# Mixing stage: the next tile turned between theta's products, gates and splits reordered, and unread products at the stage's start

## The chip, the cores and the metric

The kernel runs on one core of a Trainium2 chip as one program. The metric is the device time of one execution in microseconds (us). The profile is that of one further execution, taken by the hardware profiler; its span runs from the first to the last recorded instruction. PE is TensorE (PEld its weight loads), DVE is VectorE, ACT is ScalarE, POOL is GpSimd, SP issues the DMAs of the hardware queue.

## The reference

Three stages follow one another: attention restricted to buckets, a mixture of experts with one expert per token, and a token-mixing layer. The change lies in the last one alone:

```python
theta = x @ w_theta                      # x: 2 x 768 tokens, 512 wide
zr, zi = x * np.cos(theta), x * np.sin(theta)
y = np.einsum('ts,bsd->btd', w_tok_r, zr) + np.einsum('ts,bsd->btd', w_tok_i, zi)
u = x + y
out = u + np.maximum(u @ w_ch, 0.0)
```

Here x is the output of the experts, scaled for each token by the probability of its expert (the gate).

## The kernel before

The mixing stage (function `mixing`) works on NC = 12 tiles of 128 tokens (T = 6 for each of two batches), each 512 wide. It starts when the experts' stage has ended on all engines, since its tiles are gathered from what the experts wrote to DRAM. Each engine has a program of its own, written out by hand, and the programs meet at semaphores. An engine works through its program strictly in order, so an instruction that waits holds everything written behind it.

For tile c the steps are these.

- POOL's `gather(c)` issues an indirect DMA that brings the rows of the tile into `x_tok` (semaphore `s_g[c]`).
- `gated(c)` multiplies the tile by its gate, in place: tiles 0 to 2 on DVE (line 1332), the others on ACT (line 1257). The gates are chained by `s_gated`: gate c follows gate c-1.
- PE's `turn_x(c)` transposes the tile into the PSUM tile `m_tp` with four products by an identity (line 1424).
- ACT's `x_high(c)` rounds it to `m_xt_hi` (line 1245), and DVE's `x_low(c)` subtracts that from the unrounded one to give `m_xt_lo` (line 1328). All products are made of three such parts: high by high, high by low, low by high.
- PE's `angles(c)` makes theta for the tile in 12 products of 128x512 (line 1435).
- ACT's `turn(c)` (line 1277) and DVE's `reduce_angle(c)` (four operations, lines 1347 to 1357) bring the angle into the range of the sine.
- ACT's `waves(c)` takes sine and cosine (lines 1283 to 1286), and POOL's `times_x(c)` multiplies them by the tile (two products, line 1227).
- ACT's `z_high(c)` and DVE's `z_low(c)` split the two results. `turn(c)` waits for `z_low(c-2)`, whose buffer it writes.

The token weights come in 12 columns of 768 KB. SP loads column i into `wt_raw` (for i = 1, 3, 5 into `w_raw`), ACT's `columns_high(i)` and DVE's `columns_low(i)` split it into `wt_hi` and `wt_lo`, and PE's `from_tile(n, s)` makes six products of column n and tile s into the PSUM tile `y` (line 1454). SP loads a buffer anew only when `columns_low` has read it.

PE's order is: theta of tiles 0 to 3, with the turns between them; then, step by step, a turn, theta of one more tile, and the products of output tiles 0 to 2 with the tiles that are ready; then output tile 3 (`tokens(3)`), theta of tile 11, output tiles 4 to 6; and at last the product by `w_ch` (`channels(n)`) between the remaining output tiles.

Two earlier stages already hold products that nothing reads: 72 of 128x128 bf16 by an identity `ident_b` at the end of routing (line 848), and 20 at the experts' start (line 1064).

Of the kernel before, what the change touches and what calls it, by code (L numbers as in the profile page):

```python
# [6 lines left out]
BF16 = mybir.dt.bfloat16  # L7
# [6 lines left out]
P = 128  # L14
# [16 lines left out]
NC = B * T  # L31
# [567 lines left out]
KD = DM // P  # L599
# [513 lines left out]
    sp.dma_start(w_raw[:], src.rearrange("(k p) n -> p k n", p=P)).then_inc(s_wraw, 16)  # L1113


def mixing(nc, ctx, w_raw, s_wraw, w_tok, w_ch, y_slots, ident, pos, gate, out):
    def sb(name, shape, dt=F32):
        return ctx.enter_context(nc.sbuf_tensor(name, shape, dt))

# [122 lines left out]
    @block.scalar  # L1242
    def _(act):
        def high(dst, src, done):
            nc.scalar.copy(dst, src).then_inc(done, 1)  # L1245

        def columns_high(i):
            n, raw = raw_of(i)
            act.wait_ge(s_wt[n], landed(i))
            if i >= 3:  # L1250
                act.wait_ge(s_y, i - 2)
            high(wt_hi[i % 3][:], raw, s_wth)

        def gated(c):
            act.wait_ge(s_g[c], 16)
            act.wait_ge(s_gated, c)
            nc.scalar.activation(x_tok[:, c, :], x_tok[:, c, :], ACT.Copy, scale=gate[:, c:c + 1]).then_inc(s_gated, 1)

        def x_high(k):
            act.wait_ge(s_tp, k + 1)  # L1260
            if 2 <= k < NC + 2:
                act.wait_ge(s_th, k - 1)
            elif k >= NC + 2:
                act.wait_ge(s_ch, k - NC - 1)
            high(xt_hi[k % 2][:], tp[k % 2][:], s_xh)

        def z_high(c):
            for at, m in enumerate((1, 0)):
                act.wait_ge(s_z, 2 * c + at + 1)
                high(z_hi[:, c, m, :], z[m][c % 2][:], s_zh)  # L1270

        def turn(c):
            q = c % 2
            act.wait_ge(s_th, c + 1)
            if c >= 2:
                act.wait_ge(s_zl, 2 * c - 2)
            nc.scalar.activation(z[0][q][:], theta[q][:], ACT.Identity, bias=rounder[:],  # L1277
                                 scale=0.15915494309189535).then_inc(s_turn, 1)

        def waves(c):  # L1280
            q = c % 2
            act.wait_ge(s_r, 4 * c + 4)
            nc.scalar.activation(z[1][q][:], angle[q][:], ACT.Sin).then_inc(s_sin, 1)  # L1283
            nc.scalar.activation(z[0][q][:], angle[q][:], ACT.Abs).then_inc(s_sin, 1)
            act.wait_ge(s_sin, 3 * c + 2)
            nc.scalar.activation(z[0][q][:], z[0][q][:], ACT.Sin, bias=half_pi[:], scale=-1.0).then_inc(s_sin, 1)

        act.wait_ge(s_wraw, 16)
        for half in range(2):
            high(wm_hi[:, 2 * half:2 * half + 2, :], w_raw[:, 2 * half:2 * half + 2, :], s_whi)  # L1290
        act.wait_ge(s_c, 2)
        nc.scalar.activation(sine[:], half_pi[:], ACT.Sin).then_inc(s_sine, 1)
        x_high(0)
        columns_high(0)
        for c in range(NC):
            if c + 1 < NC:
                x_high(c + 1)
            if c >= 2:
                z_high(c - 2)
            if c == 0:  # L1300
                columns_high(1)
            turn(c)
            if c + 3 < NC:
                gated(c + 3)
            if c >= 1:
                waves(c - 1)
            if c == 1:
                columns_high(2)
            if c >= 9:
                columns_high(c - 6)  # L1310
        z_high(NC - 2)
        waves(NC - 1)
        columns_high(6)
        z_high(NC - 1)
        act.wait_ge(s_wraw, 32)
        act.wait_ge(s_th, NC)
        high(wm_hi[:], w_raw[:], s_whi)
        for i in (7, 8, 9):
            columns_high(i)
        for n in range(NC):  # L1320
            x_high(NC + n)
            if n in (1, 3):
                columns_high(10 + n // 2)

    @block.vector
    def _(dve):
# [36 lines left out]
        def columns_low(i):  # L1363
            dve.wait_ge(s_wth, i + 1)
            low(wt_lo[i % 3][:], raw_of(i)[1], wt_hi[i % 3][:], s_wtl)
# [12 lines left out]
        gated(0)  # L1378
        x_low(0)
        gated(1)  # L1380
        columns_low(0)
        gated(2)
        for c in range(NC):
            if c + 1 < NC:
                x_low(c + 1)
            if c >= 9:
                add_x(c - 9)
            if c == 1:
                columns_low(1)
            if c >= 2:  # L1390
                z_low(c - 2)
            reduce_angle(c)
            if c == 2:
                columns_low(2)
            if c >= 9:
                columns_low(c - 6)
        z_low(NC - 2)
# [20 lines left out]
    @block.tensor  # L1418
    def _(pe):
        PARTS = ((0, 0), (0, 1), (1, 0))  # L1420

        def transpose(src, k):
            for d in range(KD):
                last = nc.tensor.transpose(tp[k % 2][:, d * P:(d + 1) * P], src[:, d * P:(d + 1) * P], ident[:])  # L1424
            last.then_inc(s_tp, 1)

        def turn_x(c):
            pe.wait_ge(s_gated, c + 1)
            transpose(x_tok[:, c, :], c)

        def project(dst, k, done):
            pe.wait_ge(s_xl, k + 1)
            for d in range(KD):
                for n, (a, w) in enumerate(PARTS):
                    last = nc.tensor.matmul(dst[:], (xt_hi, xt_lo)[a][k % 2][:, d * P:(d + 1) * P],  # L1435
                                            (wm_hi, wm_lo)[w][:, d, :], start=d == 0 and n == 0,
                                            stop=d == KD - 1 and n == 2)
            last.then_inc(done, 1)

        def angles(c):  # L1440
            if c == 0:
                pe.wait_ge(s_wlo, 2)
            if c >= 2:
                pe.wait_ge(s_r, 4 * c - 4)
            project(theta[c % 2], c, s_th)

        def from_tile(n, s):

            c = n // T * T + s
            for m in (1, 0):  # L1450
                if n % T == 0:
                    pe.wait_ge(s_zl, 2 * c + 2 - m)
                for k, (a, w) in enumerate(PARTS):
                    last = nc.tensor.matmul(y[n % 4][:], (wt_hi, wt_lo)[a][n % 3][:, m, s, :],  # L1454
                                            (z_hi, z_lo)[w][:, c, m, :], start=s == 0 and m == 1 and k == 0,
                                            stop=s == T - 1 and m == 0 and k == 2)
            if s == T - 1:
                last.then_inc(s_y, 1)

        def tokens(n):  # L1460
            columns_done(pe, n)
            if n >= 4:
                pe.wait_ge(s_u, n - 3)
            for s in range(T):
                from_tile(n, s)

        def turn_u(n):
            pe.wait_ge(s_u, n + 1)
            transpose(x_tok[:, n, :], NC + n)

        def channels(n):
            if n == 0:
                pe.wait_ge(s_wlo, 3)
                pe.wait_ge(s_r, 4 * NC)
            if n >= 2:
                pe.wait_ge(s_o, n - 1)
            project(ch[n % 2], NC + n, s_ch)

        turn_x(0)
        angles(0)  # L1480
        turn_x(1)
        turn_x(2)
        angles(1)
        turn_x(3)
        angles(2)
        turn_x(4)
        angles(3)

        for s in range(T + 2):
            for n in range(3):  # L1490
                if s == n:
                    columns_done(pe, n)
                if 0 <= s - n < T:
                    from_tile(n, s - n)
            if s + 4 < NC - 1:
                turn_x(s + 5)
                angles(s + 4)
        tokens(3)
        angles(NC - 1)
        tokens(4)  # L1500
        tokens(5)
        tokens(6)
        turn_u(0)
        turn_u(1)
        tokens(7)
        for n in range(NC):
            channels(n)
            if n + 2 < NC:
                turn_u(n + 2)
            if n % 2 == 1 and n < 8:  # L1510
                tokens(8 + n // 2)


def build(nc, qT, kT, v, proj, w_gate, w_local, w1, w2, w_theta, w_tok, w_ch, out):
# [3 lines left out]
    with ExitStack() as whole:  # L1518
        def sb(name, shape, dt=F32):
            return whole.enter_context(nc.sbuf_tensor(name, shape, dt))  # L1520

        ident = sb("ident", [P, P])
        pos = sb("pos", [P, NC], U32)
        gate = sb("gate", [P, NC])
        chunk_tab = sb("chunk_tab", [P, 2, E], I32)
# [4 lines left out]
        with ExitStack() as tokens:  # L1530
# [2 lines left out]
            zeros = routed.enter_context(nc.sbuf_tensor("zeros", [P, DM], F32, side="right"))  # L1533
            x_in = tokens.enter_context(nc.sbuf_tensor("x_in", [P, 2, DM], F32))
            first = tokens.enter_context(nc.sbuf_tensor("first", [P, GATHERED], U32))
            ident_b = tokens.enter_context(nc.sbuf_tensor("ident_b", [P, P], BF16))
            s_first = tokens.enter_context(nc.semaphore("s_first"))
            s_xin0 = [tokens.enter_context(nc.semaphore(f"s_xin0{j}")) for j in range(2)]
            s_rows = tokens.enter_context(nc.semaphore("s_rows"))
# [29 lines left out]
                experts(nc, ctx, w1, w2, x_all, x_rows, x_in, s_xin0, first, s_first, y_out, pos, x_slots, s_clear, y_slots, ident, ident_b, chunk_tab, weights,  # L1569
                        lambda sp: load_w(sp, w_raw, s_wraw, w_theta))  # L1570
        with ExitStack() as ctx:
            mixing(nc, ctx, w_raw, s_wraw, w_tok, w_ch, y_slots, ident, pos, gate, out)


# [31 lines left out]
```

## Time and profile before

| what | value |
|---|---|
| time, median of 3 runs | 684.49 us (684.07, 684.49 and 687.66) |
| time of the profiled execution | 687.27 us |
| its span | 685.4 us |
| PE busy | 632.1 us (92%) |
| DVE busy | 401.0 us (59%) |
| ACT busy | 356.1 us (52%) |
| POOL busy | 250.0 us (36%) |
| mean granted TensorE clock | 0.968 of full speed |

The profiled execution took 1.9 us more than its span. Each run's time is that of the whole program; a granted clock of 1.00 is 2.4 GHz and one of 0.50 is 1.2 GHz. In the mixing stage all times below count from the start of the span; the stage begins at about 488 us.

### The profile page before, as it was taken

The numbers are of one execution on the slowest core, as the hardware profiler recorded it, in microseconds if no ns is written. First come the engines' busy times: TensorE is split into PE (matmuls) and PEld (weight loads), VectorE is DVE, ScalarE is ACT, GpSimd is POOL, SyncE is SP. The second block draws the span as 40 slices with busy tenths as digits, with TensorE's granted clock in tenths as the row PEclk, the third lists the DMA queues.
The fourth block names the chain that finished last, engine by engine and source line by source line (L and its number), as shares of the span: only waits on it lengthen the run. The fifth ranks groups of instructions, "written<-read, shape, count | busy, mean of one in ns | idle before, by whom it ended". The sixth has DMA issues, their size and how long they took to land. (4 is left out here: it accounts for less than half of the span.)

```text
span 685.4 us, 10625 instructions
## 1 busy us (share of the span) xinstructions
PE 632.1 (92%) x3781; PEld 501.6 (73%) x3782; DVE 401.0 (59%) x730; ACT 356.1 (52%) x534; POOL 250.0 (36%) x205
## 2 busy tenths in 40 slices
PE   3899999999999996699999999989479999999998
PEld 1666667767666664598899889979357888878886
DVE  6767777777877754774454344421378777732422
ACT  3776776776776772553365345421266775430200
POOL 5752708163452000287652464250335442200000
PEclk8899999999999999699999999999789999999999
DMA  9203351708163603797976676510462002422201
GB/s 292 92 1 95 144 177 62 254 8 262 39 224 112 227 11 88 264 374 261 364 263 216 231 233 202 179 63 1 157 218 87 17 1 93 153 93 55 85 31 61
DMA packets 57280, 99.24 MB, mean 145 GB/s; under 512 B 17040, under 2 KB 23184, under 8 KB 57232
## 3 DMA queue, kind: packets, MB, share of 16 engines
q1 hardware_dynamic: 54704, 90.47, 39.1%
q0 software_dynamic: 2240, 7.34, 3.0%
q10 hardware_dynamic: 288, 0.79, 0.3%
q8 instruction: 30, 0.49, 0.3%
q14 instruction: 18, 0.15, 0.1%
HBM read 69.23 MB, written 29.36 MB: 144 GB/s over the span
## 5 line engine op out<-in xcount | busy, mean ns | idle before, releaser
L396 DVE TENSOR_REDUCE scores<-scores 128x1 f32<-128x768 f32 x96 | 92.8, 966 | 41.9 <-PE scores L514 40.5
L337 ACT COPY probs_t<-turned 128x768 f32<-128x768 f32 x96 | 76.8, 800 | 63.2 <-PE turned L523 62.9
L345 ACT ACTIVATE probs<-scores,bias,scale 128x768 f32<-128x768 f32 x96 | 95.4, 993 | 12.8 <-DVE bias L403 12.4
L958 POOL TENSOR_TENSOR w_lo<-stage,w_hi 128x1024 fp32r<-128x1024 f32 x28 | 77.4, 2795 | 66.0 <-ACT w_hi L953 63.0
L523 PE MATMUL turned<-ident,probs 128*128 128x128 f32 x576 | 80.4, 276 | 5.0 <-ACT probs_t L337 5.0
L523 PEld LDWEIGHTS turned<-ident,probs 128*128 128x128 f32 x576 | 67.9, 142 | 14.2 <-issue 11.5
L1079 PE MATMUL up<-xt_hi,w_hi 128*128 128x256 f32 x256 | 73.4, 287 | 4.7 <-issue 3.2
L1079 PE MATMUL up<-xt_lo,w_hi 128*128 128x256 f32 x256 | 73.0, 285 | 0.0
L1079 PE MATMUL up<-xt_hi,w_lo 128*128 128x256 f32 x256 | 73.0, 285 | 0.0
L535 PE MATMUL pv<-probs_t,v_in 128*64 128x384 f32 x384 | 72.1, 498 | 0.0
L514 PE MATMUL scores<-k_aug,q_aug 76*128 76x384 f32 x192 | 59.8, 393 | 8.0 <-DVE k_aug L389 5.6
L514 PEld LDWEIGHTS scores<-k_aug,q_aug 76*128 76x128 f32 x192 | 29.3, 193 | 46.2 <-issue 35.3
L953 ACT CAST w_hi<-stage 128x1024 fp32r<-128x1024 f32 x56 | 56.3, 1046 | 4.2 <-DMA stage<-in_w 4.2
L1003 ACT ACTIVATE ht_hi<-up 128x512 fp32r<-128x512 f32 x32 | 19.1, 597 | 74.1 <-PE up L1079 74.1
L1454 PE MATMUL y<-z_hi,wt_hi 128*128 128x512 f32 x144 | 56.7, 394 | 0.0
L1454 PE MATMUL y<-z_lo,wt_hi 128*128 128x512 f32 x144 | 56.2, 391 | 0.0
L1454 PE MATMUL y<-z_hi,wt_lo 128*128 128x512 f32 x144 | 56.1, 390 | 0.0
L1079 PEld LDWEIGHTS up<-xt_hi,w_hi 128*128 128x128 f32 x256 | 49.1, 192 | 5.9 <-issue 4.1
L1095 PE MATMUL down<-w_hi,ht_hi 128*128 128x512 f32 x128 | 51.0, 399 | 0.0
L1032 DVE SCALAR_TENSOR_TENSOR ht_lo<-up,ht_hi 128x512 fp32r<-128x512 f32 x32 | 22.1, 691 | 48.8 <-ACT ht_hi L1003 48.8
L514 PE MATMUL scores<-k_lh,q_hl 128*128 128x384 f32 x192 | 50.5, 344 | 0.0
L1227 POOL TENSOR_TENSOR z<-z,x_tok 128x512 f32<-128x512 f32 x24 | 32.7, 1384 | 48.6 <-ACT z L1283 48.6
(185 smaller groups left out, 1282.5 us busy)
## 6 DMA issues: line engine op xcount, KB each, us to landing
stage<-in_w SPq DMA_DIRECT2D x64, 512.0 KB, 4.7
x_slots<-zeros SPq DMA_DIRECT2D x7, 1024.0 KB, 8.4
y_slots<-zeros SPq DMA_DIRECT2D x7, 1024.0 KB, 10.3
wt_raw<-in_w_tok SPq DMA_DIRECT2D x9, 768.0 KB, 4.4
q_raw<-in_qT SPq DMA_DIRECT2D x16, 384.0 KB, 5.4
k_raw<-in_kT SPq DMA_DIRECT2D x14, 384.0 KB, 6.1
x_in<-x_slots SPq DMA_DIRECT2D x8, 512.0 KB, 6.0
y_slots<-y_out SPq DMA_DIRECT2D x16, 256.0 KB, 4.9
```

The source lines that it names most:

```text
L337: nc.scalar.copy(probs_t[j % 2][:, a, :, t % 3 * P:(t % 3 + 1) * P].rearrange("k (b n) q -> k b n q", b=2), turned[:, :, 0:HALF].rearrange ...
L345: nc.scalar.activation(probs[g % 3][:].rearrange("p (b n) -> p b n", b=2), scores[g % 2][:, :, 0:HALF], ACT.Exp, bias=bias[:, pair, a, t:t ...
L396: nc.vector.tensor_reduce(neg_max[g % 2], scores[g % 2][:, :, 0:HALF], AX.XY, ALU.max, negate=True).then_inc(s_neg, 1)
L514: last = nc.tensor.matmul(scores[g % 2][:, half, 0:HALF], qq[:, rows], kk[:, half * HALF:half * HALF + HALF], start=n == 0, stop=n == 1)
L523: last = nc.tensor.transpose(turned[:, k // 3, k % 3 * P:(k % 3 + 1) * P], probs[g % 3][:, k * P:(k + 1) * P], ident[:])
L535: last = nc.tensor.matmul(pv[a * D:(a + 1) * D, 0:HALF], v_in[pair % 2][:, a, k, :], probs_t[j % 2][:, a, k, :], start=k == 0, stop=k == T ...
L953: nc.scalar.copy(w_hi[w][:, r, :], stage[:, r, :]).then_inc(s_wh, 1)
L958: name.tensor_tensor(w_lo[w][:, r, :], stage[:, r, :], w_hi[w][:, r, :].bitcast(F32), ALU.subtract).then_inc(done, 1)
L1079: last = nc.tensor.matmul(up[f // 2][:, f % 2, :], (w_hi, w_lo)[b][w][:, k, f * P:(f + 1) * P], (xt_hi, xt_lo)[a][:, k, :], start=k == 0 a ...
L1095: last = nc.tensor.matmul(down[j][:], (ht_hi, ht_lo)[a][:, f, j * P:(j + 1) * P], (w_hi, w_lo)[b][w][:, NP // 2 + f // 2, (f % 2) * DM:(f ...
L1227: nc.gpsimd.tensor_tensor(z[m][c % 2][:], z[m][c % 2][:], x_tok[:, c, :], ALU.mult).then_inc(s_z, 1)
L1454: last = nc.tensor.matmul(y[n % 4][:], (wt_hi, wt_lo)[a][n % 3][:, m, s, :], (z_hi, z_lo)[w][:, c, m, :], start=s == 0 and m == 1 and k == ...
```

## The change

In ACT's program `gated(3)` and `x_high(1)` go ahead of everything that concerns columns. Inside the loop `x_high(c+2)` stands behind `turn(c)`, where `x_high(c+1)` stood ahead of it; `gated(c+4)` stands behind `waves(c-1)`, where `gated(c+3)` stood ahead of it. `columns_high(0)` stands behind `turn(0)`, and `columns_high(1)` and `(2)` at the end of c = 1 and 2. DVE's program follows: `gated(2)` and `x_low(1)` ahead of the loop, `x_low(c+2)` behind `reduce_angle(c)`, and `columns_low(0)`, `(1)`, `(2)` at the end of c = 1, 2, 3. In PE's program `turn_x(c+1)` stands amid the 12 products of `angles(c)` for c = 0 to 3. PE's program begins with 48 unread 128x128 bf16 products and has 16 more between `turn_x(0)` and `angles(0)`; `ident_b` is kept until the kernel's end for them. The arithmetic that is read is the same.

```diff
@@ mixing, ACT @@
         x_high(0)
-        columns_high(0)
+        gated(3)
+        x_high(1)
         for c in range(NC):
-            if c + 1 < NC:
-                x_high(c + 1)
             if c >= 2:
                 z_high(c - 2)
+            turn(c)
             if c == 0:
-                columns_high(1)
-            turn(c)
-            if c + 3 < NC:
-                gated(c + 3)
+                columns_high(0)
+            if c + 2 < NC:
+                x_high(c + 2)
             if c >= 1:
                 waves(c - 1)
-            if c == 1:
-                columns_high(2)
+            if c + 4 < NC:
+                gated(c + 4)
+            if c in (1, 2):
+                columns_high(c)
             if c >= 9:
                 columns_high(c - 6)
@@ mixing, DVE @@
         gated(0)
         x_low(0)
         gated(1)
-        columns_low(0)
         gated(2)
+        x_low(1)
         for c in range(NC):
-            if c + 1 < NC:
-                x_low(c + 1)
             if c >= 9:
                 add_x(c - 9)
-            if c == 1:
-                columns_low(1)
             if c >= 2:
                 z_low(c - 2)
             reduce_angle(c)
-            if c == 2:
-                columns_low(2)
+            if c + 2 < NC:
+                x_low(c + 2)
+            if c in (1, 2, 3):
+                columns_low(c - 1)
             if c >= 9:
                 columns_low(c - 6)
@@ mixing, PE @@
-        def project(dst, k, done):
+        def project(dst, k, done, between=None):
             pe.wait_ge(s_xl, k + 1)
             for d in range(KD):
+                if d == KD // 2 and between is not None:
+                    between()
...
+        def keep_clock(times):
+            for n in range(times):
+                nc.tensor.matmul(y[3][:, 0:P], ident_b[:], ident_b[:], start=True, stop=True)
+
+        keep_clock(48)
         turn_x(0)
-        angles(0)
-        turn_x(1)
-        turn_x(2)
-        angles(1)
-        turn_x(3)
-        angles(2)
-        turn_x(4)
-        angles(3)
+        keep_clock(16)
+
+        for c in range(4):
+            angles(c, lambda: turn_x(c + 1))
```

## Rows read from the trace of the kernel before

**Rows 1.** Busy time by stretch: engines (instructions), granted clock, DMA share, GB/s.

```profile
492.00:521.36 29.36, 21.19 (x79) 16.14 (x79) 20.66 (x26) 16.41 (x24) 14.77 (x12) 0.79 0.51 179
521.36:600.00 78.64, 78.64 (x358) 65.12 (x359) 57.89 (x77) 50.84 (x78) 29.18 (x23) 1.00 0.22 74
```

**Rows 2.** Chain that ended last, a piece of it: start, us, what.

```profile
603.60 4.18 DMA wt_raw<-in_w_tok
```

**Rows 3.** Timeline of PE: start, us, line, operands [idle before <-releaser].

```profile
280.73 6.73 PE L848 MATMUL banks<-ident_b 128*128 128x128 bf16 x72
...
459.37 0.38 PE L1079 MATMUL up<-xt_hi,w_hi 128*128 128x256 f32 x1 [1.81 <-issue]
...
492.77 1.12 PE L1424 MATMUL m_tp<-ident,x_tok 128*128 128x128 f32 x4 [8.22 <-DVE x_tok L1332]
495.38 0.77 PE L1435 MATMUL theta<-wm_hi,m_xt_hi 128*128 128x512 f32 x1 [1.49 <-DVE m_xt_lo L1328]
...
500.64 0.85 PE L1424 MATMUL m_tp<-ident,x_tok 128*128 128x128 f32 x4
...
502.89 0.50 PE L1435 MATMUL theta<-wm_hi,m_xt_hi 128*128 128x512 f32 x1 [0.42 <-DVE m_xt_lo L1328]
...
521.36 0.47 PE L1435 MATMUL theta<-wm_hi,m_xt_hi 128*128 128x512 f32 x1 [1.60 <-DVE m_xt_lo L1328]
...
561.93 0.60 PE L1424 MATMUL m_tp<-ident,x_tok 128*128 128x128 f32 x4
...
566.50 0.39 PE L1454 MATMUL y<-z_hi,wt_hi 128*128 128x512 f32 x1
```

**Rows 4.** Short stretches where PE's granted clock changes or holds, columns as in rows 1.

```profile
463.50:464.00 0.50, 0.50 (x6) 0.50 (x5) 0.00 (x0) 0.00 (x0) 0.00 (x0) 0.90 0.00 0
...
487.50:488.00 0.50, 0.00 (x0) 0.00 (x0) 0.00 (x0) 0.00 (x0) 0.00 (x0) 0.50 0.00 0
...
501.00:501.50 0.50, 0.49 (x4) 0.25 (x2) 0.50 (x2) 0.00 (x0) 0.00 (x0) 0.85 1.02 385
```

**Rows 5.** DMA issued between 492.7 and 492.8 us (tile 3's gather): us to landing.

```profile
x_tok<-y_slots,pos POOLq DMA_INDIRECT x1, 7.4
```

**Rows 6.** Timeline of POOL.

```profile
561.21 2.56 POOL L1227 TENSOR_TENSOR z<-z,x_tok 128x512 f32<-128x512 f32 x2 [4.24 <-ACT z L1283]
```

**Rows 7.** Timeline of ACT.

```profile
503.38 0.69 ACT L1277 ACTIVATE z<-theta,rounder 128x512 f32<-128x512 f32 x1
503.96 0.72 ACT L1257 ACTIVATE x_tok<-x_tok,gate 128x512 f32<-128x512 f32 x1
...
556.65 0.59 ACT L1245 CAST m_xt_hi<-m_tp 128x512 fp32r<-128x512 f32 x1 [1.10 <-PE m_tp L1424]
557.14 1.14 ACT L1245 CAST z_hi<-z 128x512 fp32r<-128x512 f32 x2
559.86 0.69 ACT L1277 ACTIVATE z<-theta,rounder 128x512 f32<-128x512 f32 x1 [1.58 <-DVE z_lo L1328]
560.44 0.62 ACT L1283 ACTIVATE z<-angle 128x512 f32<-128x512 f32 x1
...
561.62 0.72 ACT L1286 ACTIVATE z<-z,half_pi 128x512 f32<-128x512 f32 x1
562.25 1.46 ACT L1245 CAST wt_hi<-w_raw 128x1536 fp32r<-128x1536 f32 x1
```

**Rows 8.** Timeline of DVE.

```profile
506.03 0.69 DVE L1357 TENSOR_SCALAR angle<-theta 128x512 f32<-128x512 f32 x1
...
517.75 2.86 DVE L1328 TENSOR_TENSOR wt_lo<-wt_raw,wt_hi 128x1536 fp32r<-128x1536 f32 x1
520.54 0.68 DVE L1328 TENSOR_TENSOR m_xt_lo<-m_tp,m_xt_hi 128x512 fp32r<-128x512 f32 x1
...
558.47 1.29 DVE L1328 TENSOR_TENSOR z_lo<-z,z_hi 128x512 fp32r<-128x512 f32 x2
...
563.74 1.76 DVE L1328 TENSOR_TENSOR wt_lo<-w_raw,wt_hi 128x1536 fp32r<-128x1536 f32 x1 [0.55 <-ACT wt_hi L1245]
```

More of the change, by code:

```diff
@@ L1113, in load_w, with mixing @@
     sp.dma_start(w_raw[:], src.rearrange("(k p) n -> p k n", p=P)).then_inc(s_wraw, 16)
-def mixing(nc, ctx, w_raw, s_wraw, w_tok, w_ch, y_slots, ident, pos, gate, out):
+def mixing(nc, ctx, w_raw, s_wraw, w_tok, w_ch, y_slots, ident, ident_b, pos, gate, out):
     def sb(name, shape, dt=F32):
@@ L1438, in project, with angles @@
             last.then_inc(done, 1)
-        def angles(c):
+        def angles(c, between=None):
             if c == 0:
@@ L1444, in angles @@
                 pe.wait_ge(s_r, 4 * c - 4)
-            project(theta[c % 2], c, s_th)
+            project(theta[c % 2], c, s_th, between)
         def from_tile(n, s):
@@ L1522, in build @@
         ident = sb("ident", [P, P])
+        ident_b = sb("ident_b", [P, P], BF16)
         pos = sb("pos", [P, NC], U32)
@@ L1535, in build @@
             first = tokens.enter_context(nc.sbuf_tensor("first", [P, GATHERED], U32))
-            ident_b = tokens.enter_context(nc.sbuf_tensor("ident_b", [P, P], BF16))
             s_first = tokens.enter_context(nc.semaphore("s_first"))
@@ L1571, in build @@
         with ExitStack() as ctx:
-            mixing(nc, ctx, w_raw, s_wraw, w_tok, w_ch, y_slots, ident, pos, gate, out)
+            mixing(nc, ctx, w_raw, s_wraw, w_tok, w_ch, y_slots, ident, ident_b, pos, gate, out)
 def kernel(**inputs):
```

## The prediction

> **What bounds the kernel now.** I read the page first: PE is busy for 92% of the span, and the chain that ended last runs through PE. Then I cut the mixing stage into stretches [rows 1]. The reader is to see two regimes. From 521.36 us PE is busy without a gap and at the full clock; from 492 to 521.36 it works for 21.19 of 29.36 us, at 0.79 of full clock on average, while DVE works for 20.66 and ACT for 16.41 us. After 521.36 the order of the changed ACT and DVE programs costs nothing as long as PE always finds its next operands. So the change is worth what it moves the moment at which PE's unbroken run begins, less any gap that it opens later. Behind theta of tile 11 the column loads follow one another through one buffer [rows 2], each started by the split of the one before; the first of them is set off by PE's products, so that whole part moves with PE.
>
> The timeline of PE [rows 3] gives the first regime: 8.22 us of nothing before the first turn at 492.77, then 1.49 us, theta of tile 0 from 495.38 to 500.64, theta of tile 1 from 502.89, and the last gap, 1.60 us, before theta of tile 4 at 521.36. The clock [rows 4] stands at 0.50 (1.2 GHz) by 487.5, 3.0 us into the long gap (it began at 492.77 - 8.22 = 484.55), and comes back at about 501.2, 5.8 us after theta's first product. So tile 0's 12 products took 5.26 us. At full clock (2.4 GHz) 18 products and a turn took 566.50 - 561.93 = 4.57 us [rows 3], about 0.23 us for a product and 2.8 for 12.
>
> **Unread products.** The nearest row is the 72 of line 848: 6.73 us, 0.093 each, most of them at the half clock [rows 3]. The 48 cost between 4.5 us (that mean) and 5.1 (were all at the half clock; 0.107 each, a product of 128 columns being a quarter of theta's 5.26/12 = 0.44), from about 488.2, so they end at 492.7 to 493.3. The first turn could start at 492.77: 0 to 0.5 us late, I take 0.4. The 16 take 1.5 to 1.7 us against a gap of 1.49: 0 to 0.2, hidden by the split of tile 0. With the clock back some 4 to 6 us after 488.2 (the restart at 459.37 [rows 3] had its full clock after 463.5 [rows 4], 4.1 us on), tile 0's theta runs at full clock: 495.8 + 2.8 + a turn of 0.4 = 499.0 instead of 500.64, with the turn of tile 1 inside it.
>
> The Trainium skill, in "TensorE: Matmul & The Clock Gate", Part 4, PE-mode transpose, says that transposes don't count as work for the clock as other products do. By that page the four of tile 0 would not carry on what the 48 began, and the clock might return only amid theta; no row here separates the two. What that would make of the time is the first rival below, worked out from rows.
>
> **What gains on PE meet on ACT.** `gated(3)` now stands ahead of `x_high(1)` and `turn(0)`. The gather of tile 3 is issued between 492.7 and 492.8 and lands 7.4 us later [rows 5], at 500.2. In the old order this landing hurt nobody, since `gated(3)` ran at 503.96 [rows 7]. Now everything on ACT waits for it. From the rows: gate 500.2 to 500.8 (0.72 long, and the next starts 0.1 before its end, as at 559.86 and 560.44), `x_high(1)` to 501.4 (0.59), `x_low(1)` to 502.1 (0.68, rows 8), theta of tile 1 at 502.3 against 502.89: only 0.6 us earlier. `turn(0)` starts at 501.3 against 503.38 [rows 7]. And PE idles from 499.0 to 502.3, 3.3 us. The long gap had cost the clock after 3.0 us, and by the restart at 459.37, after 1.81 us idle, it went too. So I expect tile 1's theta mostly at the half clock. At full clock it and the turn inside end at 505.5, all at half (5.26 + 1.12) at 508.7; with the clock back about 5 us on, 507.3. I take that.
>
> **What gains on DVE.** Up to `x_low(4)` the old DVE program holds `columns_low(1)` and `(2)` (the latter 2.86 us, stretched beside POOL's products [rows 8], alone 1.76), the new one only `columns_low(0)`, which the old had ahead. So `x_low(4)` should be done earlier. Forward from 507.3: `turn(1)` 507.3 to 508.0; `reduce_angle(1)` 2.6 us (tile 0's took that: `turn(0)` ended at 503.38 + 0.69 = 504.1 [rows 7], the last of the four at 506.03 + 0.69 = 506.7 [rows 8]) to 510.6; `x_low(3)` to 511.2; `columns_low(0)` stretched to 2.2, 513.4; the two `z_low(0)` wait for POOL's 2.56 us of products, which wait for the waves of tile 0, now behind tile 3's `x_high` (509.6), and for their `z_high` behind `columns_high(1)`, and end near 516.0; `turn(2)` and `reduce_angle(2)` to 519.2; `x_low(4)` to 519.9. Theta of tile 4 starts at 520.05, 1.3 us earlier than 521.36. But `columns_low(1)` and `z_low(1)` are still to come: 1.8 (2.2 beside POOL) + 1.3 us, to 523.3, while PE is through with theta of tile 4 at 522.8; then `turn(3)`, 0.7, the reduction 2.5 and `x_low(5)` 0.6 give 527.2 for tile 5, where 521.36 plus 12 products, 12 products and a turn is 527.2 too. So the early gain is spent by then: -1.4 if the clock had held at tile 1, 0 as worked out, +1.5 where the gap of about 2.9 us ahead of theta of tile 4 takes the clock once more. I take +0.5. POOL's later gathers and SP's column loads start later than before (the loads behind `columns_low(0)`, some 12 us later), but the first use of column 2 is later by more than a load takes.
>
> **A gap that the loop opens later.** In steps 4 to 8 of the loop ACT and DVE have room, as PE has 30 products and a turn for each step. At step 9 they haven't. Old order: `x_high(10)` 556.65, both `z_high(7)` at once, `turn(9)` 559.86, waves, `columns_high(3)` 562.25 [rows 7], `columns_low(3)` 563.74 to 565.50 [rows 8]; PE starts output tile 3 at 566.50 [rows 3], 1.0 us of slack. New order: `x_high(10)` still can't start before 556.65, since it waits for the turn that PE makes there, and now `waves(7)` stands behind it. Sine at 557.1, done 557.75; POOL's two products 2.56 us [rows 6] to 560.3; the second `z_high(7)` 0.62 to 560.95; `z_low` 0.7 to 561.65; `turn(9)` 561.7, 1.8 late. Then `x_high(11)` stands ahead of the waves and waits for the turn ending at 562.53 (561.93 + 0.60 [rows 3]): to 563.0; waves 1.8 (560.44 to 562.25 [rows 7]) to 564.8; `columns_high(3)` 1.46 to 566.3; `columns_low(3)` 1.76 to 568.1; PE at 568.2. Late next: output tile 3 by 1.7 us, and with it everything behind. Bounds 1.2 to 2.2; nothing covers it, since PE has no other instruction ahead.
>
> **Sum.** +0.5 + 1.7 = +2.2 us (rounded up by 0.1 for the products at the start that delay tile 0's turn). Against the profiled execution's own 687.27 us (span 685.4 and 1.9 around it) that is 689.6. That execution lies 2.8 over the median; the other two agree at 684.1 and 684.5, and a lost clock stretch or two would make such a difference. So I put the sum on the median: 684.5 + 2.3 = 686.8.
>
> **Rivals.**
> 1. The gap before tile 1 costs no clock, or the clock comes back only amid tile 0's theta, so that PE is busy to 501 and there is no gap. Then tile 1's theta ends near 505.5, the early part gives 1.4, the late gap takes 1.7: 684.8. For it: how the clock goes varies with the start. Against: 3.3 us idle is more than the 3.0 after which it went.
> 2. Faster: tile 3's rows land by about 497.5, as they would with a landing time of 4.7 instead of 7.4 us. Then ACT isn't held, `turn(0)` starts at 499.0, PE's gap is 0.6 us, the clock stays, and the DVE chain moves by 3 us or more; with the late gap partly closed, 680.5. Decides below about 498. Against: only loads that the change doesn't move lie beside these gathers.
> 3. Slower: the clock falls again in the gap before theta of tile 4 and in that before output tile 3, each followed by 3 to 5 us at half clock in the part where PE sets the end, 1.5 us each in addition: 690. It decides where a gap grows over about 1.8 us (1.81 at 459.37 cost the clock, 1.60 at 521.36 did not); mine are 2.9 and 1.7.
> 4. No effect: the DVE program is the bound and its work is the same; 684.5, told from rival 1 by the gaps alone, and counted with it.
>
> **How the numbers follow.** Forecast (686 to 688) 0.48, rivals 1 and 4 0.20, rival 2 0.12, rival 3 0.20. 0.5% is 3.4 us, about what a measurement of this kernel can tell from no change: below 681.1 faster, above 687.9 slower. Faster: rival 2, 0.12. Slower: rival 3 and the upper third of the forecast's own spread, 0.35. Same: 0.53. The range reaches from most of rival 2 left out (681.3) to rival 3 taken in (690.5); the forecast's own is 685.3 to 688.5.
>
> **What would show it.** Right: `gated(3)` on ACT starts at the landing of tile 3's rows near 500, with ACT idle ahead of it; PE idle some 3 us between theta of tiles 0 and 1; a granted clock of 0.50 over part of tile 1's theta; theta of tile 4 within 1.5 us of 521; a gap of 1.2 to 2.2 us before output tile 3, ended by `wt_lo`. Wrong: `gated(3)` without a wait, theta of tile 5 before 525, or PE unbroken from tile 4 to tile 11. All of it would be wrong, too, if the stage began elsewhere than at 488.

## The result and the profile after

The changed kernel took 688.83 us (median of 20 runs, 684.69 to 694.98) against 686.3 us for the kernel before (20 runs, 683.89 to 689.29). The ratio is 1.0041, with a 95% interval of 1.0024 to 1.0058: 1.6 to 4.0 us slower. One of the 20 runs, the one of 694.98 us, was in a slower state and doesn't count in the ratio. The two medians are 2.5 us apart. The forecast was +2.3 us on a base of 684.5, the median of three runs; over 20 runs the kernel before has its median 1.8 us higher. So the time itself, 688.83, lies 2.0 us above the forecast 686.8.

The profiled execution after has a span of 688.0 us against 685.4. Its mixing stage began at 486.58 (DVE's first memset of the stage) instead of 488.13, 1.55 us earlier, though the instructions ahead of it are the same. Over all traces of this document that start lies between 486.40 and 489.07, and it doesn't follow the edits. So times are compared below from the stage's start: 201.4 us to the span's end against 197.3, 4.1 us more.

First PE's timeline, the answers to [rows 3]: start, us, line, operands, idle time ahead and what ended it.

```profile
486.55 4.18 PE L1482 MATMUL y<-ident_b 128*128 128x128 bf16 x48 [3.55 <-PEq L1571]
491.25 0.66 PE L1423 MATMUL m_tp<-ident,x_tok 128*128 128x128 f32 x4 [0.51 <-DVE x_tok L1333]
491.74 1.06 PE L1482 MATMUL y<-ident_b 128*128 128x128 bf16 x16
493.40 0.47 PE L1436 MATMUL theta<-wm_hi,m_xt_hi 128*128 128x512 f32 x1 [0.60 <-DVE m_xt_lo L1329]
...
500.54 0.80 PE L1436 MATMUL theta<-wm_hi,m_xt_hi 128*128 128x512 f32 x1 [3.70 <-DVE m_xt_lo L1329]
...
519.44 0.47 PE L1436 MATMUL theta<-wm_hi,m_xt_hi 128*128 128x512 f32 x1 [2.71 <-DVE m_xt_lo L1329]
...
567.92 0.51 PE L1455 MATMUL y<-z_hi,wt_hi 128*128 128x512 f32 x1 [1.52 <-DVE wt_lo L1329]
...
614.45 0.47 PE L1436 MATMUL theta<-wm_hi,m_xt_hi 128*128 128x512 f32 x1 [1.76 <-DVE m_xt_lo L1329]
```

The reader sees what the unread products buy (theta of tile 0 starts at 6.8 us of the stage instead of 7.3 and runs at full clock) and how it is idled away: 3.70 us with nothing ahead of theta of tile 1. Then come 2.71 us before tile 4, a gap of 1.52 before output tile 3 that the old order didn't have, and 1.76 before the product by `w_ch` (0.73 in the kernel before, seen in its timeline at 611.82).

ACT's timeline says who held PE. The answers to [rows 7] follow.

```profile
498.57 0.72 ACT L1257 ACTIVATE x_tok<-x_tok,gate 128x512 f32<-128x512 f32 x1 [6.04 <-DMA x_tok<-y_slots,pos]
499.19 0.56 ACT L1245 CAST m_xt_hi<-m_tp 128x512 fp32r<-128x512 f32 x1
499.66 0.69 ACT L1277 ACTIVATE z<-theta,rounder 128x512 f32<-128x512 f32 x1
...
556.39 0.59 ACT L1245 CAST m_xt_hi<-m_tp 128x512 fp32r<-128x512 f32 x1 [1.30 <-PE m_tp L1423]
556.87 0.64 ACT L1283 ACTIVATE z<-angle 128x512 f32<-128x512 f32 x1
...
560.24 0.62 ACT L1245 CAST z_hi<-z 128x512 fp32r<-128x512 f32 x1 [0.62 <-POOL z L1227]
561.68 0.69 ACT L1277 ACTIVATE z<-theta,rounder 128x512 f32<-128x512 f32 x1 [0.82 <-DVE z_lo L1329]
...
564.61 1.46 ACT L1245 CAST wt_hi<-w_raw 128x1536 fp32r<-128x1536 f32 x1
```

ACT stood 6.04 us at `gated(3)`, until tile 3's rows had landed; `x_high(1)` and `turn(0)`, which don't need them, stood behind. At 556 one sees the second mechanism: the sine of tile 7 starts only behind the `x_high(10)` that waits for PE, POOL's products come after it, and `columns_high(3)` ends at 566.07.

The clock by stretch (columns as in [rows 1]), to be read against [rows 4]:

```profile
499.50:500.00 0.50, 0.00 (x0) 0.00 (x0) 0.21 (x1) 0.50 (x2) 0.00 (x0) 0.64 0.96 361
500.00:506.00 6.00, 5.46 (x15) 4.39 (x16) 3.59 (x6) 2.92 (x4) 0.00 (x0) 0.50 0.07 25
...
519.44:524.00 4.56, 4.56 (x13) 3.63 (x14) 3.71 (x5) 3.28 (x6) 2.60 (x2) 0.63 0.36 97
```

It fell at 499.6, 2.8 us into the 3.70 us gap, and was back at about 506.5, so nearly all of tile 1's theta ran at 1.2 GHz. It fell again at about 520.1, after the 2.71 us gap, and came back at 523.5.

The kernel before has such a second fall too, which neither the rows nor the prediction show: after a gap of 2.47 us before theta of tile 3 its clock went to 0.50 at about 514.7 and came back at about 518.2 (PE's timeline, then the clock by stretch).

```profile
513.36 0.47 PE L1435 MATMUL theta<-wm_hi,m_xt_hi 128*128 128x512 f32 x1 [2.47 <-DVE m_xt_lo L1328]
...
515.00:518.00 3.00, 3.00 (x9) 2.35 (x8) 2.67 (x5) 2.97 (x7) 1.53 (x2) 0.50 0.00 0
```

So the second fall isn't a loss that only the changed kernel has.

### The profile page after: what moved, and what is told of

Read it like the earlier page. It is cut to its first block and busy times, and to the rows that moved or that the text cites. A ratio compares the mean times of both kernels' runs of the same rounds, so it can differ in the third digit from the quotient of the medians.

```text
span 688.0 us, 10753 instructions
## 1 busy us (share of the span) xinstructions
PE 635.3 (92%) x3845; PEld 504.1 (73%) x3846; DVE 399.4 (58%) x730; ACT 356.3 (52%) x534; POOL 251.1 (36%) x205
## 5 line engine op out<-in xcount | busy, mean ns | idle before, releaser
L345 ACT ACTIVATE probs<-scores,bias,scale 128x768 f32<-128x768 f32 x96 | 95.3, 993 | 13.1 <-DVE bias L403 12.6
L1095 PE MATMUL down<-w_lo,ht_hi 128*128 128x512 f32 x128 | 50.2, 392 | 0.0
```

Source lines behind the costliest of these rows:

```text
L345: nc.scalar.activation(probs[g % 3][:].rearrange("p (b n) -> p b n", b=2), scores[g % 2][:, :, 0:HALF], ACT.Exp, bias=bias[:, pair, a, t:t ...
L1095: last = nc.tensor.matmul(down[j][:], (ht_hi, ht_lo)[a][:, f, j * P:(j + 1) * P], (w_hi, w_lo)[b][w][:, NP // 2 + f // 2, (f % 2) * DM:(f ...
```

## The experiments

The twelve kernels of the experiments ran in groups, each group beside its own runs of the kernel before. The table gives the ratio to that kernel with its 95% interval. It also gives three readings of the one profiled execution: the start of the last `turn` (tile 11) and the end of the span, both in us from the stage's start, and how long the load of column 9 took to land (DMA view and chain).

| kernel | ratio (95%) | last turn | span's end | column 9 |
|---|---|---|---|---|
| before | 1 | 89.5 | 197.3 | 4.18 |
| changed | 1.0041 (1.0024 to 1.0058) | 92.6 | 201.4 | 5.38 |
| e1 no unread products | 1.0042 (1.0018 to 1.0067) | 90.1 | 198.1 | 4.30 |
| e2 gate of tile 3 later | 1.0028 (1.0004 to 1.0053) | 87.6 | 196.6 | 5.35 |
| e3 late order | 1.0035 (1.0016 to 1.0053) | 87.9 | 197.4 | 5.90 |
| e4 both orders | 1.0008 (0.9984 to 1.0031) | 85.8 | 196.5 | 5.29 |
| e5 unread products alone | 1.0013 (0.9990 to 1.0035) | 87.9 | 196.9 | 5.42 |
| e6 load later | 1.0041 (1.0019 to 1.0062) | 88.5 | 199.4 | 5.75 |
| e7 wide products | 1.0035 (1.0016 to 1.0055) | 90.4 | 198.2 | 4.07 |
| e8 both orders, wide | 0.9982 (0.9962 to 1.0003) | 87.7 | 195.8 | 4.24 |
| e9 turns amid theta alone | 0.9991 (0.9966 to 1.0016) | 90.2 | 198.0 | 4.15 |
| e10 wide products alone | 0.9994 (0.9971 to 1.0017) | 90.1 | 198.0 | 4.26 |
| e11 e8 with the load later | 0.9984 (0.9965 to 1.0003) | 90.7 | 198.7 | 4.25 |
| e12 e11, columns behind | 0.9955 (0.9935 to 0.9974) | 87.7 | 195.3 | 4.03 |

The interval of a ratio spans some 3 us, so differences of 1 us between two kernels aren't told apart by the times; the traces show the mechanism, each in one execution with its own luck with the clock. Nor is the traced execution always a typical one: it took 1.0 us more than the median in the changed kernel (689.86) and in the one before (687.27), but 1.8 less in e6, 1.2 less in e7 and 2.6 more in e11.

**e1, without the unread products.**

```diff
-        keep_clock(48)
         turn_x(0)
-        keep_clock(16)
```

> The changed kernel without its 48 and 16 unread products. Theory A (the gate of tile 3 ahead of x_high(1) holds ACT until its rows land, so the clock won for tile 0's theta is idled away before tile 1's): tile 0's theta runs at 1.2 GHz and ends only shortly before x_low(1) is ready, PE's gap before theta of tile 1 is under 1.5 us in place of 3.7, tile 1's theta runs at full clock; the time is 1 to 1.5 us below that of the changed kernel, a ratio to before of 1.002. Theory B (the unread products pay, the order alone costs): tile 0's theta is 2.5 us late and everything after it with it, 690 to 691 us, a ratio of 1.007.

```profile
502.43 0.50 PE L1436 MATMUL theta<-wm_hi,m_xt_hi 128*128 128x512 f32 x1 [0.51 <-DVE m_xt_lo L1329]
```

The gap before tile 1's theta is 0.51 us in place of 3.70, that theta begins 13.9 us into the stage (14.0 in the changed kernel), and the last turn comes 2.5 us earlier. The time didn't follow: 1.0042 beside 1.0041. Theory B's ratio of 1.007 lies just above the interval, and the 1 to 1.5 us of theory A weren't found either, though its ratio of 1.002 lies at the interval's lower end. So the 64 products are worth nothing measurable in this order, one way or the other.

**e2, e3 and e4, the two orders.** e2 moves one gate:

```diff
         x_high(0)
-        gated(3)
         x_high(1)
...
             if c == 0:
+                gated(3)
                 columns_high(0)
```

> The changed kernel with gated(3) behind turn(0) on ACT instead of ahead of x_high(1). Theory A: x_high(1) follows the turn of tile 1 at once, PE's gap before theta of tile 1 falls from 3.7 us to under 1, the clock holds, turn(0) starts some 2 us earlier from the stage's start; 2 to 3 us gained against the changed kernel, a ratio to before of 1.000 to 1.001. Theory C (DVE's work sets when PE's unbroken run begins, whatever ACT waits for): theta of tile 5 starts no earlier, less than 0.7 us gained, ratio 1.003 to 1.004.

e3 moves the waves and columns ahead of `x_high` from c = 8 on, with DVE to match:

```diff
@@ ACT @@
-            if c + 2 < NC:
+            if c < 8:
                 x_high(c + 2)
...
             if c >= 9:
                 columns_high(c - 6)
+            if 8 <= c < NC - 2:
+                x_high(c + 2)
@@ DVE @@
-            if c + 2 < NC:
+            if c < 9:
                 x_low(c + 2)
...
+            if c == 9:
+                x_low(c + 2)
```

> The changed kernel with waves(c-1) and the columns ahead of x_high(c+2) from c = 8 on, and columns_low(3) ahead of x_low(11) on DVE. Theory A (late gap of 1.5 us before output tile 3 comes from waves(7) and waves(8) standing behind x_highs that wait for PE's turns): the gap is gone, 1.5 us gained, ratio to before 1.002. Theory D (the gap only takes up time that the column loads behind it would cost anyway): the gap is gone, PE's gap before the product by w_ch grows instead, nothing gained, ratio 1.004.

e4 is both edits.

> Both of the edits before this one together on the changed kernel. Theory A: the gains add up, 3.5 to 4.5 us under the changed kernel, ratio to before 0.998 to 0.999. Theories C and D: ratio 1.003 to 1.004.

In e2 the gap before tile 1's theta is gone (under 0.25 us) and `turn(0)` starts at 10.3 us of the stage instead of 13.1, the last one at 87.6 instead of 92.6. Theta of tile 5 begins at 35.5 us instead of 40.4, so theory C falls in the trace. Of the 5.0 us at the last turn some is the clock's: in this execution it didn't fall again once it was back. The ratio, 1.0028, lies between the two forecasts, and its interval reaches into both; why the times show so much less than the trace stays open. ACT's timeline shows what is left of the mechanism: the wait for the landing, shorter now, stands ahead of `x_high(2)`, and PE waits 1.53 us before theta of tile 2.

```profile
499.88 0.72 ACT L1257 ACTIVATE x_tok<-x_tok,gate 128x512 f32<-128x512 f32 x1 [0.84 <-DMA x_tok<-y_slots,pos]
500.51 1.46 ACT L1245 CAST wt_hi<-wt_raw 128x1536 fp32r<-128x1536 f32 x1
501.88 0.57 ACT L1245 CAST m_xt_hi<-m_tp 128x512 fp32r<-128x512 f32 x1
```

In e3 the gap before output tile 3 is gone, as theory A says; but the gap before the product by `w_ch` grew from 1.76 to 2.46 us. That is theory D's mark, but most of it is the load of column 9, which itself took 0.5 us longer in this trace. The interval holds theory A's 1.002 as well as D's 1.004. In e4 both gains show in the trace (last turn 85.8, 6.8 us earlier than in the changed kernel), and 1.9 us of them were given back by the end. The wait before the product by `w_ch` was 2.07 us there, and the clock fell behind it:

```profile
612.00:614.00 2.00, 2.00 (x6) 1.52 (x6) 0.00 (x0) 0.00 (x0) 0.00 (x0) 0.50 0.48 197
```

In the times e4 is 0.33% under the changed kernel by the two ratios, 2.3 us of the 3.5 to 4.5 expected.

**What lay on the late load.** The chains of the first traces showed a thing that the prediction had no term for. The load of column 9 took 4.18 us in the kernel before and 5.38 after; in the stretch of that load the DMA view of the changed kernel has a second queue:

```profile
q1 hardware_dynamic: 144, 0.79, 39.3%
q8 instruction: 1, 0.02, 1.0%
issues: line engine op xcount, KB each, median us to landing
wt_raw<-in_w_tok SPq DMA_DIRECT2D x1, 768.0 KB, 5.4
```

One packet of instructions was fetched there; beside this load there was none in the kernel before and in e1. e5, e7 and e10 test it with the orders held fixed. e5 is the kernel before plus the two calls of `keep_clock`.

> The kernel before plus the 48 and 16 unread products alone, all orders as before. Theory A: tile 0's theta ends at full clock some 10.5 us after the stage's start in place of 12.5, but ACT stands at columns_high(0) until its load lands (10 us) and at columns_high(1) (13 us), so turn(0) starts only about 1 us earlier than its 15.2; and, theory F (128 more PE instructions move a fetch of instructions onto the third of the late column loads, which in the four traces with unread products so far, the changed kernel's among them, took 5.3 to 5.9 us, in the two without 4.2 to 4.3), about 1 us is given back at the load for column 9: ratio 1.000, 0.998 to 1.002. Theory B (the unread products are what pays): 2 us or more gained, ratio below 0.997.

e7 and e10 make the unread work from a quarter of the products, each four times as wide, on the changed kernel and on the one before:

```diff
-                nc.tensor.matmul(y[3][:, 0:P], ident_b[:], ident_b[:], start=True, stop=True)
+                nc.tensor.matmul(y[3][:], ident_b[:], ident_b[:].unsqueeze(1).to_broadcast([P, 4, P]), start=True, stop=True)
...
-        keep_clock(48)
+        keep_clock(12)
         turn_x(0)
-        keep_clock(16)
+        keep_clock(4)
```

> The changed kernel with the unread products made of 12 and 4 of 512 columns instead of 48 and 16 of 128: the same time on PE, 96 instructions fewer. Theory F: the 31st fetch of instructions is gone (or moved), the load of column 9 takes 4.2 to 4.5 us instead of 5.4, PE's gap before the product by w_ch falls from 1.8 us to about 0.8; 1 us gained, ratio to before 1.002 to 1.003. Rival H (the slow third load is chance or comes of the clock or the order): it stays over 5 us, ratio 1.004.

> The kernel before with 12 and 4 unread products of 512 columns (the fifth run with wide products). Theory F (a fetch of instructions falls on the load for column 9 where PE has 128 more instructions): the load takes 4.1 to 4.5 us where the fifth run's took 5.4, the gap before the product by w_ch is under 1.2 us where it was 1.85, ratio 0.996 to 0.999 (the fifth run's 1.0013 less some 1 us and what the clock gives). Rival H (chance): over 5 us, ratio 1.000 to 1.002.

The chain of e7:

```profile
604.90 4.07 DMA wt_raw<-in_w_tok
```

Over all kernels of the table, the six with 64 narrow products (changed, e2 to e6) have an instruction packet beside the load of column 9, and it took 5.29 to 5.90 us; the eight others have none, and it took 4.03 to 4.30. The gap before the product by `w_ch` is 1.76 to 2.46 us in the six and 0.51 to 1.04 in the eight. So theory F holds in the traces, and rival H falls. The count of fetches was still 31 with the wide products, against 30 without any: the fetch went elsewhere, it didn't go away. Around the stage's start it lies at 3.3 to 4.1 us of the stage with the narrow products and at 8.9 to 11.6 with the wide ones, beside the first column loads; the late one lies at 113 to 121 us with the narrow ones and at 126 to 129 with the wide ones, behind column 9.

When a fetch meets a load, the moment counts. In the six traces it began 1.0 to 2.8 us after the load of column 9. In the kernel before, one began 3.5 us after the load of column 7, and that load took 4.22 us, like any other; in e7, e8, e10, e11 and e12 one began 0.3 to 0.6 us ahead of the load of column 7, and it took 4.19 to 4.43. In the times the 1 us isn't resolved: e7 1.0035 against 1.0041, e10 0.9994 against e5's 1.0013. e5 also shows that the unread products don't pay in the old order: `turn(0)` came 1.8 us earlier (13.4), and the ratio is 1.0013 with an interval that starts at 0.9990, not below 0.997; theory B falls.

**e6, the landing.**

```diff
             if i == 0:
-                sp.wait_ge(s_g[0], 16)
+                sp.wait_ge(s_g[3], 16)
```

> The changed kernel with SP's first column load (and so the second) waiting for the rows of tile 3 instead of tile 0. Theory A (the two loads of 768 KB beside the gathers make tile 3's rows land 7.3 us after their issue): they land 3.5 to 5 us after it, ACT's wait at gated(3) ends 2.5 us or more earlier, PE's gap before theta of tile 1 is under 1.5 us; the columns come some 3 to 4 us later, which columns_high(0) behind turn(0) feels by 1 to 2 us; 1 to 2.5 us gained on the changed kernel, ratio to before 1.000 to 1.003. Rival G (POOL's own making of the descriptors sets the landing): still 7 us, nothing gained, 1.004 or more.

Tile 3's rows landed 3.9 us after their issue instead of 7.3 (DMA view, first line), and ACT was through at 8.5 us of the stage instead of 12.0:

```profile
x_tok<-y_slots,pos POOLq DMA_INDIRECT x1, 3.9
...
494.94 0.72 ACT L1257 ACTIVATE x_tok<-x_tok,gate 128x512 f32<-128x512 f32 x1 [1.78 <-DMA x_tok<-y_slots,pos]
```

The two others with this wait, e11 and e12, have 3.7 us; the eleven kernels without it have 6.9 to 9.1. So the two column loads beside the gathers make the landing late, and rival G falls. PE's gap before tile 1's theta was under 0.25 us, that before tile 2's 1.24, behind an ACT that now waited 1.19 us for column 0. The last turn came 4.1 us earlier, but only 2.0 us were left at the span's end: column 9 took 5.75 us, PE waited 2.27 before the product by `w_ch`, and the clock fell behind that gap (0.50 from 612 to 614). The time didn't move at all, 1.0041; the traced execution was 1.8 us below the median, so its 2.0 us may be no more than that. Where the gain of the early part went in the timed executions stays open.

**e9, PE's part alone**: the loop `for c in range(4): angles(c, lambda: turn_x(c + 1))` in the kernel before.

> The kernel before with PE's part alone: turn_x(c+1) amid the products of angles(c) for c = 0 to 3, no unread products, ACT's and DVE's orders as before. Tile 0's theta is made at half clock and now ends 0.9 us later by the turn inside it; turn(0) on ACT waits for columns_high(1) (15.2 us after the stage's start) anyway. Theory A (ACT and DVE set the pace here, PE's order is free): turn(11) within 0.7 us of its 89.5, ratio 1.000, 0.998 to 1.002. Rival I (the turns ahead of theta were what kept PE waiting): 1.5 us or more gained, ratio under 0.998.

Measured 0.9991, last turn 90.2, 0.7 us later and not 1.5 earlier: in the trace PE's order is free here, as theory A says. The interval, 0.9966 to 1.0016, doesn't shut out rival I's 0.998.

**e8, e11 and e12, towards a better version.** e8 is e4 with the wide products.

> The changed kernel with gated(3) behind turn(0), the late order (waves and columns ahead of x_high from c = 8 on), and the 12 and 4 wide unread products. Theories A and F: turn(11) starts 86 us after the stage's start (89.5 in the kernel before), the load of column 9 takes 4.2 to 4.5 us, so 2.5 to 3.5 us under the kernel before, ratio 0.995 to 0.997. If the late loads set the end whatever comes before (theory D): ratio 0.999 to 1.001.

e11 adds e6's wait.

> The eighth run (gate of tile 3 behind turn(0), late order, wide products) with SP's first column load waiting for tile 3's rows. Theory A (in the eighth run ACT still stood 2.1 us at gated(3), now ahead of x_high(2), and PE 2.75 us before tile 2's theta): that wait is gone, tile 2's theta starts 1.5 to 2.5 us earlier; the column loads come 4 us later and cost up to 1 us of it; ratio to before 0.995 to 0.998. Rival (DVE's work up to x_low(4) and the late loads set the end): the wait is gone but theta of tile 5 is no earlier, ratio 0.998 to 0.999.

e8 came out at 0.9982, between the two forecasts; column 9 took 4.24 us, but the last turn was at 87.7 where 86 was expected, with 2.75 us of idle PE before tile 2's theta. Tile 3's rows landed 9.1 us after their issue here, against 7.2 in e4. e11 gave 0.9984, and missed: the wait at the gate was gone, and its place was taken by the column that stood next to it, 3.66 us, with PE idle for 4.3 us before tile 2's theta:

```profile
498.63 0.71 ACT L1257 ACTIVATE x_tok<-x_tok,gate 128x512 f32<-128x512 f32 x1
503.00 1.47 ACT L1245 CAST wt_hi<-wt_raw 128x1536 fp32r<-128x1536 f32 x1 [3.66 <-DMA wt_raw<-in_w_tok]
504.38 0.58 ACT L1245 CAST m_xt_hi<-m_tp 128x512 fp32r<-128x512 f32 x1
```

That load of column 0 took 7.39 us, where with the same wait of SP in e6 it took 4.43. The same loads and gathers lie beside it in both, but in e11 a fetch of instructions too, begun 0.9 us after the load; in e6, with the narrow products, the fetch had come ahead of it.

```profile
495.58 7.39 DMA wt_raw<-in_w_tok
...
q8 instruction: 1, 0.02, 0.9%
```

In e12 it was 7.22 us, again with a fetch, 0.5 us after its start. So what the wide products spared column 9 came back, with this wait, at column 0.

e12's edit takes the column out of ACT's way:

```diff
             if c == 0:
                 gated(3)
-                columns_high(0)
...
-            if c in (1, 2):
-                columns_high(c)
+            if c in (1, 2, 3):
+                columns_high(c - 1)
```

> The eleventh run with columns_high(0), (1), (2) at the end of c = 1, 2, 3 on ACT, so that no load stands ahead of x_high(2). Theory A (each wait for data from DRAM that stands ahead of an x_high on ACT is paid by PE): ACT waits for no landing between 11 and 17 us after the stage's start, PE's gap of 4.3 us before theta of tile 2 falls below 1.5 us, turn(1) and turn(2) come 2 to 4 us earlier than in the eleventh run (18.2, 28.8), and turn(11) at 85 to 88 against 90.7; ratio to before 0.995 to 0.997. Rival C (DVE's work up to x_low(4) sets the pace): the gap is gone, turn(11) stays at 88 or later, ratio 0.998.

```profile
499.48 0.71 ACT L1257 ACTIVATE x_tok<-x_tok,gate 128x512 f32<-128x512 f32 x1
500.97 0.59 ACT L1245 CAST m_xt_hi<-m_tp 128x512 fp32r<-128x512 f32 x1 [0.78 <-PE m_tp L1426]
501.45 0.72 ACT L1257 ACTIVATE x_tok<-x_tok,gate 128x512 f32<-128x512 f32 x1
502.37 0.69 ACT L1277 ACTIVATE z<-theta,rounder 128x512 f32<-128x512 f32 x1 [0.19 <-PE theta L1439]
```

ACT waits for no landing there any more. PE's timeline:

```profile
502.96 0.47 PE L1439 MATMUL theta<-wm_hi,m_xt_hi 128*128 128x512 f32 x1 [0.64 <-DVE m_xt_lo L1330]
...
516.60 0.47 PE L1439 MATMUL theta<-wm_hi,m_xt_hi 128*128 128x512 f32 x1 [2.56 <-DVE m_xt_lo L1330]
...
609.74 0.47 PE L1439 MATMUL theta<-wm_hi,m_xt_hi 128*128 128x512 f32 x1 [0.51 <-DVE m_xt_lo L1330]
```

The gap before tile 2's theta is 0.64 us, `turn(1)` comes at 14.3 us instead of 18.2, `turn(2)` at 24.5 instead of 28.8, the last at 87.7 instead of 90.7. The time is 683.35 against 686.02, ratio 0.9955 (0.9935 to 0.9974): 1.8 to 4.5 us under the kernel before, the fastest of all. What it keeps is the 2.56 us before theta of tile 4, which every kernel with the new order shows (2.56 to 2.72): there DVE's chain to `x_low(4)` ends last, so rival C names a true bound, only a later one. Its interval stands clear of the changed kernel's, 1.0024 to 1.0058, so the times, too, show that the changed kernel can be mended, but for all the repairs together (orders, landing and wide products) and for none of them alone.

## Why the prediction was right, step by step

The direction, the size and the class (within 0.5%, towards slower) came out, and the main steps are in the trace. One term was missing, one was too small, and luck had a part in two.

- **Unread products.** Forecast 4.5 to 5.1 us for the 48 and a first turn up to 0.5 us late; they took 4.18 us, since the clock came back at about 489.4, 2.9 us after they began, and the turn wasn't late. That is luck of the execution: in e3 the same 48 took 5.28 us, with the clock back after 6.0, and the first turn came 0.4 us late as forecast. Over the eleven traces with unread products the clock came back after 2.8 to 3.3 us in five and after 5.4 to 6.0 in six. Theta of tile 0 ran at full clock and ended some 2 us earlier in the stage than before (last product at 496.44, 9.9 us in). What the Trainium skill says of transposes in "TensorE: Matmul & The Clock Gate", Part 4, PE-mode transpose, no run here tests: in the changed kernel the clock was back before the first of them, and in the six traces with the late return it came back amid them, close behind the unread products.
- **ACT held by tile 3's rows.** Forecast: landing 12.0 us into the stage (500.2), ACT idle up to it, PE idle 3.3 us. Measured 12.0 and 3.70 us. e6 shows that the landing is late because of the two column loads, and e2 that it is the order which makes PE pay for it.
- **The clock in that gap.** Forecast back 5 us after the restart, measured 6.0. `turn(1)` at 20.2 us of the stage where 19.2 was expected: this term was mis-sized by 1.0 us. That the clock fell at all was in part luck. e7 has the same orders and a gap of 3.43 us before theta of tile 1, and the clock held at 1.00 all through. Its theta of tile 5 began at 38.3 us, 0.8 earlier than in the kernel before; the prediction gives 1.4 earlier for this case.

```profile
499.50:508.00 8.50, 4.98 (x23) 3.79 (x24) 4.60 (x8) 5.04 (x7) 0.00 (x0) 1.00 0.33 124
```

The prediction also misread its own nearest row: at the restart at 459.37 the clock was still at 1.00 and fell only at about 460.2, 0.8 us into the new products.
- **DVE's gain.** Forecast theta of tile 4 1.3 us earlier than in the kernel before; measured 32.9 us into the stage against 33.2, 0.4 us earlier, and the 0.9 us between are those of `turn(1)`. The spread of the early part was given as -1.4 to +1.5; theta of tile 5 started at 40.4 (after the turn at 526.63) against 39.1, so it came to +1.3 where +0.5 was taken. The second fall of the clock, after the 2.71 us gap, is in it: rival 3's mechanism, at one of its two places. At the other, the 1.52 us gap, the clock held. Rival 3's 1.8 us doesn't decide it: in the nine traces with a gap of 2.71 or 2.72 us before theta of tile 4 the clock fell in six and held in three (e2, e4, e7).
- **The late gap.** Forecast 1.7 us (1.2 to 2.2), ended by `wt_lo`; measured 1.52, ended by `wt_lo`. e3 removes it with the order alone.
- **The missing term.** From output tile 3 on the prediction moved everything as one block. The load of column 9 took 1.2 us longer, PE's gap before the product by `w_ch` grew by 1.0 us, and what goes with it is the longer program of PE, not its order: 128 more instructions put a fetch amid that load.

From the stage's start the profiled execution thus lost 1.3 + 1.5 + 1.0, with 0.3 in small pieces the 4.1 us; the ratio of the timed runs, +2.8 us, is nearer to the +2.3 forecast. Part of that nearness is luck: the trace's own sum is larger, and one execution differs from the next in how the clock falls (e7, of the same order, has its last turn 2.2 us earlier). Rival 1's first form (the gap costs no clock) is e7's trace; its ratio of 1.0035 isn't the 684.8 us of that rival, which is no change. Rival 2's landing is e6, and it did not bring 680.5: 689.47 us were measured. That the columns, which then land later, take back part of what the earlier landing brings is seen in e11's trace (3.66 us of waiting) and, smaller, in e6's (1.19).

## What to carry to other kernels

When work is moved ahead on an engine that runs in order, look up when the data of everything now standing in front lands: a gate that nobody waited for had PE idle for 3.7 us once `x_high(1)` stood behind it, and each repair merely showed the next landing until all three were behind (e2, e11, e12). A turn that waits for PE doesn't belong ahead of work that feeds PE's next wait. Instructions added only for the clock are also code to fetch: fewer of them don't do away with the fetch but move it, so look in the DMA view at what it falls beside (column 9 with the narrow products, column 0 with the wide ones in e11). And before a clock term is trusted, look at it in more than one trace.

## What was not expected of the hardware

- A single packet of instructions of 0.02 MB beside a load of 768 KB went with 5.29 to 5.90 us to landing in place of 4.03 to 4.30, in six traces of six against eight of eight. The load of column 0 shows it again, this time with the wide products: 7.39 and 7.22 us in e11 and e12 with a fetch amid it, against 4.43 in e6, of the narrow ones, without. Fetches at the very start or end of a load of the same size left it at 4.19 to 4.43. That the packet itself delays the load is the nearest reading; no run adds a fetch and nothing else.
- The clock came back 2.9 us after the start of the 48 unread products in the changed kernel and 6.0 us after it in e3, with the same products; theta's own start in the kernel before needed 5.8 us, and the restart after the 3.70 us gap 6.0 us.
- It fell amid work: 0.7 us after PE had restarted at 519.44 in the changed kernel, 1.3 us after the restart at 513.36 in the one before.
- An indirect DMA of 128 rows landed after 3.9 us with only other gathers beside it, and after 7.3 us with two loads of 768 KB as well (e6 against the changed kernel; 3.7 to 3.9 in three traces, 6.9 to 9.1 in eleven).
